# Attention and two gated layers on one core: VectorE's, ScalarE's and GpSimd's order at a layer's end and in a layer's first group

## The reference, cut to what matters

```python
def reference(**kwargs):
    attn_out = _attn_ref(q, k, v)        # 4 batches, 8 heads, 576 positions, head size 64,
                                         # window of 128, a bias that falls with distance, softmax
    x = attn_out.transpose(0, 2, 1, 3).reshape(B * S, H * D)          # 2304 x 512
    x = 1 / (1 + exp(-(x @ w_gate))) * (x @ w_val) @ moe_w_out        # d_ff 1536
    return ((x @ w1) * (x @ w2) @ w3) @ moe2_w_out                    # d_ff 1024
```

## Time and profile before

| | |
|---|---|
| median of 3 runs | 885.34 us (883.81 to 888.36) |
| the profiled execution | 886.31 us, of which the span of its instructions is 884.5 us |
| TensorE busy | 864.6 us, 98% of the span, 5272 matmuls |
| VectorE busy | 515.2 us, 58% |
| ScalarE busy | 475.0 us, 54% |
| GpSimd busy | 594.9 us, 67% |
| DMA | 78.79 MB, mean 89 GB/s |
| granted TensorE clock | 0.9 of full in the second to fourth of 40 slices, 1.0 in all later ones |

### The profile page before, as it was taken

The page is one execution under the profiler, slowest core; times in us unless marked ns, Lnnn a source line. Parts: engine busy times, 40 slices in busy tenths (PEclk is TensorE's granted clock), DMA queues, the critical chain, the costliest instruction groups (busy, mean ns, idle before and its releaser), DMA issues.

```text
span 884.5 us, 15389 instructions
## 1 busy us (share of the span) xinstructions
PE 864.6 (98%) x5272; PEld 825.7 (93%) x5272; DVE 515.2 (58%) x1209; ACT 475.0 (54%) x1043; POOL 594.9 (67%) x502
## 2 busy tenths in 40 slices
PE   5999999999999999999999999999999999999998
PEld 4887899999999999999999999999999999999998
DVE  5464656555467646656456656555676555576554
ACT  5566575666655644668555575633544444445330
POOL 3449588666655986758766663896859866738930
PEclk8999999999999999999999999999999999999999
DMA  8465323304222133331332122222221222212202
GB/s 243 123 197 161 113 93 103 92 15 117 91 79 82 35 104 98 100 126 52 96 109 88 48 81 80 72 72 72 80 102 46 84 72 72 72 49 72 72 24 73
DMA packets 59453, 78.79 MB, mean 89 GB/s; under 512 B 23152, under 2 KB 40688, under 8 KB 59376
## 3 DMA queue, kind: packets, MB, share of 16 engines
q1 hardware_dynamic: 58432, 77.52, 27.8%
q10 hardware_dynamic: 944, 0.30, 0.1%
HBM read 70.98 MB, written 6.82 MB: 88 GB/s over the span
## 4 chain that ended last, share of the span: by engine, by line
PE 80%; DVE 4%; ACT 4%; POOL 4%; issue 3%; DMA 2%; SPq 1%; ACTq 0%; DVEq 0%; POOLq 0%
PE quad_ps L610 14%; PE quad_ps L612 13%; PE quad_ps L611 13%; PE o_ps L610 11%; PE o_ps L612 10%; PE o_ps L611 10%; PE attn_ps L668 4%; PE attn_ps L633 3%; PE attn_ps L648 2%; DMA wo_lo_raw<-w_out 1%; DVE h_lo L1071 1%; PE quad_ps L633 1%; PE quad_ps L648 1%; POOL wq_lo L1280 1%; POOL wq_lo L1273 1%
## 5 line engine op out<-in xcount | busy, mean ns | idle before, releaser
L610 PE MATMUL quad_ps<-xs_hi,wq_hi 128*128 128x384 f32 x840 | 291.6, 347 | 3.2 <-DVE quad_ps L1043 1.8
L612 PE MATMUL quad_ps<-xs_hi,wq_lo 128*128 128x384 f32 x840 | 281.5, 335 | 0.0
L611 PE MATMUL quad_ps<-xs_lo,wq_hi 128*128 128x384 f32 x840 | 281.3, 335 | 0.0
L610 PE MATMUL o_ps<-h_hi,wo_hi 128*128 128x384 f32 x480 | 166.3, 347 | 3.0 <-DVE h_lo L1071 2.4
L610 PEld LDWEIGHTS quad_ps<-xs_hi,wq_hi 128*128 128x128 f32 x840 | 157.8, 188 | 10.3 <-issue 3.9
L612 PE MATMUL o_ps<-h_hi,wo_lo 128*128 128x384 f32 x480 | 161.3, 336 | 0.0
L611 PE MATMUL o_ps<-h_lo,wo_hi 128*128 128x384 f32 x480 | 161.1, 336 | 0.0
L611 PEld LDWEIGHTS quad_ps<-xs_lo,wq_hi 128*128 128x128 f32 x840 | 158.0, 188 | 0.0
L612 PEld LDWEIGHTS quad_ps<-xs_hi,wq_lo 128*128 128x128 f32 x840 | 157.7, 188 | 0.0
L1236 POOL TENSOR_TENSOR soft<-soft,recip 128x384 f32<-128x384 f32 (+2 forms) x80 | 58.3, 729 | 145.4 <-DVE recip L985 145.3
L1280 POOL TENSOR_TENSOR wq_lo<-wsum,wq_hi 128x1024 fp32r<-128x1024 f32 x60 | 144.3, 2405 | 8.5
(11 more groups left out here) (68 smaller groups left out, 1365.4 us busy)
## 6 DMA issues: line engine op xcount, KB each, us to landing
raw_q<-w SPq DMA_DIRECT2D x24, 512.0 KB, 3.7
raw_q<-w_gate SPq DMA_DIRECT2D x18, 512.0 KB, 3.6
raw_q<-w_val SPq DMA_DIRECT2D x18, 512.0 KB, 4.6
wo_lo_raw<-w_out SPq DMA_DIRECT2D x18, 512.0 KB, 4.2
wo_lo_raw<-w_times_wout SPq DMA_DIRECT2D x12, 512.0 KB, 3.8
w_raw<-w3t SPq DMA_DIRECT2D x16, 256.0 KB, 3.2
outT<-xf SPq DMA_DIRECT2D x8, 384.0 KB, 3.8
q_sb<-qT SPq DMA_DIRECT2D x30, 96.0 KB, 3.5
```

Of the source, the lines that this page charges most:

```text
L610: pe.matmul(out, lh, rh, start=start, stop=False, skip_group_check=onto)
L611: pe.matmul(out, lh, rl, start=False, stop=False, skip_group_check=onto)
L612: return pe.matmul(out, ll, rh, start=False, stop=stop, skip_group_check=onto)
```

## The change

The sums, products and copies are the same before and after, on the same engines; only their order on VectorE and ScalarE changes, and one wait of GpSimd. There are five edits.

1. VectorE, val section of a layer's last group: `hidden_lo(g, C12)` goes ahead of `result_21` and `hidden(g, C21)`.
2. VectorE, val section of a layer's first group: the reciprocal of the softmax step goes from ahead of `hidden(g, C11)` and `result_22` to behind them.
3. ScalarE, gate section of a first group: `out_hi(g)` goes from ahead of the three gates to behind them.
4. ScalarE, val section of a first group: the high part of the next group's plain blocks (now `plain_hi`) goes ahead of the gate of C21 and of `keep`; that of the sums (`sums_hi`) stays where it was.
5. GpSimd, gate section of a first group: it waits for P4's input to be split, and no longer for P3's, ahead of its part of the softmax step and `weight_sums(g + 1, 0)`.

```diff
-            def weights_hi(g, m):
+            def plain_hi(g, m):
                 act.wait_ge(rawq_in[m], 16 * (g + 1))
                 wait(act, prod_done, 14 * g - 7 * (1 - m))
                 nc.scalar.copy(wq_hi[m][:, 0:PLAIN], raw_q[m][:, GW:GW + PLAIN]).then_inc(wq_hi_done[m], 1)
+            def sums_hi(g, m):
                 act.wait_ge(wsum_done[m], 4 * (g + 1))
+                wait(act, prod_done, 14 * g - 7 * (1 - m))
                 nc.scalar.copy(wq_hi[m][:, PLAIN:7 * GW], wsum[m][:, :]).then_inc(wq_hi_done[m], 1)
...
                 elif kind == "val":
+                    if first_of(g):
+                        plain_hi(g + 1, 0)
                     gate(g, C21)
                     keep(2 * g + 1)
...
                 if kind == "val" and first_of(g):
-                    weights_hi(g + 1, 0)
+                    sums_hi(g + 1, 0)
...
                 if kind == "gate":
-                    out_hi(g)
+                    if not first_of(g):
+                        out_hi(g)
                     gate(g, C11)
                     if m is not None and m % 2:
                         out_copies(m)
                     gate(g, C22)
                     gate(g, C12)
+                    if first_of(g):
+                        out_hi(g)
...
                     sums_26(2 * g + 1)
-                    if n is not None:
+                    if n is not None and not first_of(g):
                         reciprocals(n)
                     hidden(g, C11)
                     result_22(2 * g + 1)
+                    if n is not None and first_of(g):
+                        reciprocals(n)
                     hidden_lo(g, C11)
                     hidden(g, C22)
                     result_12(2 * g + 1)
                     hidden(g, C12)
                     hidden_lo(g, C22)
+                    if last_of(g):
+                        hidden_lo(g, C12)
                     result_21(2 * g + 1)
                     if last_of(g):
                         hidden(g, C21)
-                        hidden_lo(g, C12)
...
-                        pool.wait_ge(xs_split[P3], inst)
+                        pool.wait_ge(xs_split[P4], inst)
```

More of the change, by code:

```diff
@@ L834, in weights_hi @@
                 nc.scalar.copy(wq_hi[m][:, 0:PLAIN], raw_q[m][:, GW:GW + PLAIN]).then_inc(wq_hi_done[m], 1)
+            def sums_hi(g, m):
                 act.wait_ge(wsum_done[m], 4 * (g + 1))
+                wait(act, prod_done, 14 * g - 7 * (1 - m))
                 nc.scalar.copy(wq_hi[m][:, PLAIN:7 * GW], wsum[m][:, :]).then_inc(wq_hi_done[m], 1)
+            def weights_hi(g, m):
+                plain_hi(g, m)
+                sums_hi(g, m)
             def out_hi(g):
```

## The result

| | before | changed |
|---|---|---|
| median | 885.16 us (883.81 to 888.36, 6 runs) | 877.38 us (876.83 to 880.15, 6 runs) |
| ratio of the changed kernel to the one before | | 0.9917, 95% interval 0.9903 to 0.9932 |
| the profiled execution, its span | 886.31 us, 884.5 us | 878.12 us, 876.3 us |

The kernel became 0.8% faster: 7.8 us by the medians, against 5.3 us forecast. On TensorE the profile has 4.1 us less busy time and the rest less waiting.

The account below looks back on a forecast made before the run. TensorE, busy 98% of the span, was taken as the bound. Terms of 2.9, 1.46, 0.48 and 0.41 us made 5.3 us off the profiled 886.31 us, 881.0 us, and a median of 880.0 us; range 878.2 to 884.2 us.

Parts of the forecast that it names:

- edit 3's term: Group 0's gate section: with w_out's cast behind the gates, TensorE's 0.21 us wait goes, winning 0.48 us with the restart.
- The wait in group 12: TensorE's other wait for a gate, not in a first group, was to stay, so nothing was counted for it.
- The restart of 0.27 us: Each TensorE wait was taken to cost about 0.27 us beyond its idle time, from group 25's pair0 against pair1.
- Edit 1's queue: VectorE in pair0: C21's sum and product move back 0.6 us; group 9 wins nothing, its wait moving on to xf.
- Rival B: The bank is late in every pair0, so the low-part move wins only 0.8 to 1.5 us: 881.5 to 882.2; chance 0.19.
- ScalarE's plain cast: First groups' val section: moved ahead of C21's gate, it only fills ScalarE's waiting and costs nothing if keep is in time.
- rival C: Gate sections of groups 1, 11 take back the 1.9 us won in groups 0, 10: 881.9 us; chance 0.14.
- the rule's estimate: Group 26: VectorE with two SBUF inputs waits until running GpSimd reading SBUF finishes, giving 0.54 us, not 0.41.
- Rival D: First groups' val sections: keep comes late behind the casts, six groups lose 8.8 us, 890.8 us; chance 0.06.
- Rivals A and E: Whole kernel: A, the terms as worked out, 880.0 us, chance 0.50; E, no visible effect, 885 us, chance 0.08.

Follow-up runs that it names:

- r7: The changed kernel without the early cast of the plain blocks: 878.5 us, ratio 0.9936 to the kernel before.
- r5: The kernel before with only VectorE's reciprocal moved behind C22's sum in first groups: 884.2 us, ratio 0.9999.
- r14: The kernel before with only ScalarE's cast of the plain blocks moved ahead of C21's gate in first groups: 883.96 us (one run).
- r15: The kernel before, unchanged, run once more: 887.01 us (one run).
- r9: Changed kernel, plus w_out's cast behind C11's gate in other groups, VectorE's pass-end input sum behind C21's low part: 878.38 us, ratio 0.9923 to the kernel before.

## Why the prediction was wrong

**The steps that failed** are terms of the sum. The largest error is edit 3's term: 0.48 us, "Bounds: 0 and 0.5", read from one wait in one execution, where the runs give 1.26 us on average. Next, edit 1 was counted by TensorE's five listed waits alone, which put group 5 and pair1 of group 9 at nothing; they gave 0.79 us. The wait in group 12, which "stays", went in every profile of the changed kernel (0.6 us), and edits 2 and 4 gave 0.2 us more than forecast. The mechanisms of edits 1, 2, 3 and 5 were as described where they had a term; that of edit 4 was not. What the runs gave:

| term | predicted | measured |
|---|---|---|
| edit 1: groups 9, 15, 19, 25, 29 | 0, 0.66, 0.6, 0.83, 0.83 | 0, 0.60, 0.59, 0.83, 0.84 |
| edit 1: group 5, pair1 of group 9 | none | 0.35, 0.44 |
| edits 2 and 4 | 1.46 | 1.7 |
| edit 3 | 0.48 | 1.26 on average, 0.51 in the pair of profiles |
| edit 5 | 0.41 | 0.42 |
| wait for the gate in group 12 | "stays" | 0.6, cause open |
| sum of the terms | 5.3 | 7.6 |

7.6 us agrees with the three ratios of the changed kernel (7.3, 8.1 and 6.9 us); without group 12 it is 7.0. The two profiles' 8.2 us holds 1.45 us from the start and group 4, by the clock and by chance.

1. **The restart of 0.27 us** on top of an idle time held within 0.06 us in every place where a wait went whole; in group 19 some 0.2 us stayed, as forecast (pair0 lasts 8.56 us there, 8.35 in group 25). That a wait costs something where none is listed was missed: I counted only the listed waits, and group 5 has one that isn't. The prediction's opening sentence that all waits lie in a layer's last or first group leaves out group 12's, which edit 3's part names.
2. **Edit 1's queue** came out as worked out, group 9's new wait for `xf` of 0.34 us included. Rival B, the bank late everywhere, was wrong: of the other four pair0 sections none waits for `xf`.
3. **Edits 2 and 4.** "ScalarE's plain cast … only fills time …; it costs nothing" was half of it. r7 and r5 show that without it rival C is true in part, and 0.65 us is given back; r14 shows that it alone cures most of the wait. Another 0.2 us was won in the gate sections of groups 1 and 11.
4. **Edit 3** was priced from one execution: the wait for a DMA was read as if it were a constant of the kernel. "Bounds: 0 and 0.5" was the wrong part; the three executions of the same kernel show 0.5, 0.6 and 2.3 us over the section with the edit, in group 0 alone. The Trainium skill's page on ScalarE's tables (ScalarE: Activation LUTs, What ACT_TABLE_LOAD costs) would have the gate 1.4 us behind the load. The sigmoid starts 0.02 us after the load's end in r15's rows above, and edit 3 gained more, not less.
5. **Edit 5** gained 0.42 us, 0.41 predicted. By the rule of the Trainium skill (SBUF — State Buffer, Who interferes with whom) it would have been 0.54. The rule itself is borne out better than my sum: four VectorE operations that fell on a running GpSimd one ended 0.81 to 0.82 us after its end, whether they took 1.36, 2.09 or 2.59 us (group 26: 792.79 against 791.97), and the same holds all over the profiles (see the last section). What the rule's estimate missed is that 0.13 of the 0.95 us passes before the wait. I used the rule for one term and never asked where else in the kernel the two engines overlap; there it was worth 0.44 us in this change and 1.06 us against r9.
6. **Rival D** did not come: no wait for `s` stands among TensorE's waits. Rivals A and E gave too little.

## What to carry to other kernels

Price a wait for a DMA from several executions, not from one: moving work from behind such a wait is worth its average, and the profile at hand may show the mildest case. Compare sections by their lengths too, not only by the listed waits, since a short idle time, or one under a modelled matmul end, is in no list. Look at the granted clock of both executions before a difference between two profiles is given to an edit. Before a VectorE operation with both inputs in SBUF is moved, look at what GpSimd does at its new place: 0.95 us can turn into 2.6, and which of the two starts first is decided by tenths of a microsecond.

## What the runs showed of the hardware

- A VectorE operation on 128x768 with both inputs in SBUF takes 0.95 us alone, and when it falls on a running GpSimd operation it ends 0.81 to 0.82 us after that one's end: 2.59 us in two places, 2.09 and 1.36 us in others. Over the eighteen profiles 227 VectorE operations of this shape took more than 0.97 us, and each of them ended 0.80 to 0.82 us after a GpSimd operation that was running when it started.
- The transfer of `w_out` in group 0 (512 KB) went from issue to the cast in 5.8 us in the kernel before and in 7.6 us in r15 (issued at 96.39, cast at 103.97), with the same instructions around it.
- The first gate section started at 95.0 to 99.1 us in profiles whose instructions up to there are the same, a spread larger than what any single edit here won. It goes with the clock granted in the first 22 us: 95.0 to 96.7 us at 1.00, 96.6 to 97.4 at 0.92 or 0.93, 98.0 to 99.1 at 0.87 to 0.89.
